# Columns of the near scores kept by place within 16, and one ScalarE placement moved ahead of another, in the two units that run before the main loop

## The chip, the core and the metric

The kernel runs on one core of a Trainium2 chip. The metric is the device time of one execution, in microseconds. Five engines work side by side and wait for each other on semaphores: TensorE (PE, with its weight loads shown as PEld), VectorE (DVE), ScalarE (ACT), GpSimd (POOL) and SyncE (SP, which here only issues DMAs).

## What is computed

Three stages, all in float32. First a gated linear attention over 4 batches, 8 heads, 768 tokens, 48 channels, written in the reference as a recurrence:

```python
for t in range(S):
    state = alpha[:, :, t, :, None] * state + np.einsum('bhd,bhe->bhde', k[:, :, t], v[:, :, t])
    y[:, :, t] = np.einsum('bhd,bhde->bhe', q[:, :, t], state)
```

Then, on the 3072 rows of 384 numbers that this gives, a feed-forward layer `elu(x @ w_in) @ w_out` with 2048 hidden channels, and last four experts of 1024 hidden channels each, `out += p_e * (relu(x @ w1[e]) @ w2[e])`, with the probabilities `p` normalised over the experts.

## The kernel before

Tokens are taken in 12 units of 256. The feed-forward and expert layers go over 6 tiles of 512 tokens in 48 steps each; every float32 product there is made of three products of rounded parts (`hi` and `lo`), so a step is 18 matmuls of 128x512. Attention for units 2 to 11 is cut into pieces that run between the steps of the tile before. Attention for units 0 and 1 (`EARLY` chunks of 128 tokens, four of them) has nothing to run beside: it stands ahead of the loop over steps, and the change touches only this part.

**Scores by levels.** Within a chunk of 128 tokens the decayed scores between tokens are made by doubling. At level `l`, with span `h = 2**l`, tokens pair up in blocks of `2h`: the queries of the right half of each block meet the keys of the left half. PE makes those scores (`early_pairs`), then DVE multiplies the right queries and left keys by their decays (`early_updates`, lines 701 and 702: the products of decays are doubled at line 710), and the next level can begin. So PE and DVE take turns within a unit, and the two units are interleaved by `EARLY_ORDER`: (unit, level) = (0,0) (0,1) (0,2) (1,0) (0,3) (1,1) (0,4) (1,2) (0,5) (1,3) (0,6) (1,4) (1,5) (1,6).

**Levels 0 to 5** are made by `early_pairs` with 64 matmuls of 64 keys by 32 right queries (line 481), keys of 64 tokens against the 32 queries of those tokens which stand to the right at this level. Every level thus gives whole 64x32 blocks, of which only some places are wanted. **Level 6** uses `level` (line 445), 32 matmuls of 64x64.

**Placing the scores.** For the spans 1, 2, 4 and 8 (`l < MASKED`) DVE copies under a mask from PSUM into `near`, a piece of the buffer `blocks` with 64 columns for each head and half (`early_masked`, line 725, two instructions a level, 256 elements each). For spans 16 and 32 the wanted places are rectangles, and ACT copies them one by one (`early_rect`, line 917: 8 copies of 16x128, or 4 of 32x256). Then ACT copies `near` into the weights of the unit (`early_near`, line 926: 2 copies of 64x1024; the weights of unit 0 are `pair_weights`, those of unit 1 stand in `p_rows`). Span 64 goes from PSUM to the weights directly (`early_rect` at level 6, line 908: 4 copies of 64x256).

**After the levels** PE turns the keys (`transpose_k`, line 500), ACT brings them to SBUF (`k_tokens`, line 933, `k_tok`), PE multiplies them with the values (`outer`, line 518), DVE adds that to the state (line 744), and `attend` (lines 542, 546, 551) gives the output of each chunk, which ACT (`x_hi`, line 959) and DVE (`x_lo`, line 756) bring to SBUF as the input of the first step. All orders are written out by hand. The lists of PE and of ACT in this part:

```python
for u, l in EARLY_ORDER[:-2]: early_pairs(u, l)
transpose_k(0); transpose_k(1); early_pairs(1, LEVELS - 2); outer(0); early_pairs(1, LEVELS - 1)
attend(0); transpose_k(2); transpose_k(3); attend(1); outer(1); attend(2); attend(3)
```

```python
early_rect(0, MASKED); early_rect(0, MASKED + 1); early_near(0)
early_rect(1, MASKED); early_rect(0, LEVELS - 1); k_tokens(0); k_tokens(1)
early_rect(1, MASKED + 1); early_near(1); early_rect(1, LEVELS - 1); k_tokens(2); k_tokens(3)
```

`outer(0)` waits for span 64 of unit 0 and, by chunk, for `k_tokens`. `attend(0)` waits for `early_near(0)`.

Of the kernel before, what the change touches and what calls it, by code (L numbers as in the profile page):

```python
# [11 lines left out]
B, HEADS, S, D = 4, 8, 768, 48  # L12
P = 128
# [3 lines left out]
HALF = P // 2  # L17
TOKENS = B * S
LEVELS = 7
LOW = 4  # L20
SUB = 1 << LOW
COL = 32
# [23 lines left out]
LEAD = 2  # L46
EARLY = 2 * LEAD
MASKED = 4
PARTS = 10

NPROD = SUB - 1
# [97 lines left out]
def program(nc, q_d, k_d, a_d, v_d, qb_d, kb_d, ab_d, k0_d, v0_d, w_d, probs_d, eye_d, masks_d, sc_d, pn_d, out):  # L149
    ctx = ExitStack()  # L150
    with ctx:
# [12 lines left out]
        QT = sbs("q_low", 2, [P, PAIRS, UNIT])  # L164
# [254 lines left out]
        def _(pe):  # L419
# [38 lines left out]
            def early_pairs(u, l):  # L458
# [15 lines left out]
                for c in range(2):  # L474
                    for pr in range(PAIRS):
                        for j in range(2):
                            t = slice(P * c + HALF * j, P * c + HALF * (j + 1))
                            for sd in range(2):
                                r = slice(HALF * sd, HALF * (sd + 1))
                                right = QT[u][r, pr, t].rearrange("p (n two h) -> p n two h", two=2, h=1 << l)[:, :, 1, :]  # L480
                                last = nc.tensor.matmul(banks[sd][HALF * j:HALF * (j + 1), COL * (PAIRS * c + pr):COL * (PAIRS * c + pr + 1)],  # L481
                                                        KL[u][r, pr, t], right, start=True, stop=True)
                last.then_inc(e_step[u], 1)
# [167 lines left out]
        def _(dve):  # L651
# [60 lines left out]
            def early_masked(u, l):  # L712

                h = 1 << l
                dve.wait_ge(e_step[u], l + 1)
                if l:
                    dve.wait_ge(e_mask[u], l)
                else:
                    dve.wait_ge(masks_in, 16)
                    dve.wait_ge(near_clear, 1)  # L720
                mask = mk[:, l, :].rearrange("p (n h) -> p n h", h=h).unsqueeze(1).broadcast_to([P, HEADS, COL // h, h])
                for sd in range(2):
                    dst = near[:, u].rearrange("p (a s) (n two h) -> p s a n two h", s=2, two=2, h=h)[:, sd, :, :, 1, :]
                    src = ps_l[l % 2][u][sd][:, 0:HEADS * COL].rearrange("p (a n h) -> p a n h", a=HEADS, h=h)
                    last = nc.vector.copy_predicated(dst, mask.bitcast(U32), src)
                last.then_inc(e_mask[u], 1)

# [153 lines left out]
        def _(act):  # L881
# [18 lines left out]
            def early_rect(u, l):  # L900
# [8 lines left out]
                else:  # L909
                    if l == MASKED:  # L910
                        act.wait_ge(e_mask[u], MASKED)
                    for sd in range(2):
                        dst = near[:, u].rearrange("p (a s) t -> p s a t", s=2)[:, sd]
                        src = ps_l[l % 2][u][sd][:, 0:HEADS * COL].rearrange("p (a t) -> p a t", a=HEADS)
                        for m in range(HALF // h):
                            rows, n = slice(2 * m * h, (2 * m + 1) * h), m % (COL // h)
                            last = nc.scalar.copy(dst[rows, :, (2 * n + 1) * h:(2 * n + 2) * h], src[rows, :, n * h:(n + 1) * h])
                last.then_inc(e_rect[u], 1)

            def early_near(u):  # L920
                act.wait_ge(e_rect[u], LEVELS - 1 - MASKED)
                act.wait_ge(cleared, CLEARS)
                w = weights[u].rearrange("p c a t -> p (c a) t")
                for m in range(2):
                    rows = slice(HALF * m, HALF * (m + 1))
                    last = nc.scalar.copy(w[rows, :, rows], near[rows, u])
                last.then_inc(e_near, 1)

            def k_tokens(g):
# [72 lines left out]
            early_rect(0, MASKED)  # L1002
            early_rect(0, MASKED + 1)
            early_near(0)
            early_rect(1, MASKED)
            early_rect(0, LEVELS - 1)
            k_tokens(0)
            k_tokens(1)
            early_rect(1, MASKED + 1)
# [204 lines left out]
```

## Time and profile before

| | before |
|---|---|
| time, median of 3 runs | 1322.0 us (1321.72 to 1322.02) |
| profiled execution | 1323.48 us, of which the span from first to last instruction is 1321.5 us |
| PE busy | 1303.8 us, 99% of the span |
| DVE, ACT, POOL busy | 64%, 46%, 40% |
| granted TensorE clock | 1.0 in every slice |

Busy shares here are for the whole span. The changed part is the first 52 us of it, and what it is worth is read there, from the instructions in order of time. A matmul's end is modelled, and matmuls overlap, so a group of matmuls starts some 0.2 us before the modelled end of the group ahead. A duration is followed in some rows by the idle time of that engine before it, and by what ended this.

### The profile page before, as it was taken

The numbers are of one execution on the slowest core, as the hardware profiler recorded it, in microseconds if no ns is written. First come the engines' busy times: TensorE is split into PE (matmuls) and PEld (weight loads), VectorE is DVE, ScalarE is ACT, GpSimd is POOL, SyncE is SP. The second block draws the span as 40 slices with busy tenths as digits, with TensorE's granted clock in tenths as the row PEclk, the third lists the DMA queues.
The fourth block names the chain that finished last, engine by engine and source line by source line (L and its number), as shares of the span: only waits on it lengthen the run. The fifth ranks groups of instructions, "written<-read, shape, count | busy, mean of one in ns | idle before, by whom it ended". The sixth has DMA issues, their size and how long they took to land.

```text
span 1321.5 us, 26259 instructions
## 1 busy us (share of the span) xinstructions
PE 1303.8 (99%) x10472; PEld 1074.5 (81%) x10472; DVE 846.1 (64%) x1129; ACT 607.8 (46%) x1051; POOL 532.6 (40%) x454
## 2 busy tenths in 40 slices
PE   6999999999999999999999999999999999999999
PEld 6787888888888888888888888888888888888887
DVE  7786767665676665576766567676557645654455
ACT  3656443357434347534336743434753433663332
POOL 1571858711655841453861175583145311100011
PEclk9999999999999999999999999999999999999999
DMA  5535353355244236336336534423623332533330
GB/s 199 177 104 174 107 185 93 96 153 186 89 137 151 76 101 198 126 108 200 89 87 169 171 91 150 144 85 93 215 98 109 100 97 87 151 96 99 101 93 31
DMA packets 84028, 165.77 MB, mean 125 GB/s; under 512 B 30146, under 2 KB 31683, under 8 KB 83908
## 3 DMA queue, kind: packets, MB, share of 16 engines
q1 hardware_dynamic: 83616, 163.97, 40.1%
q8 instruction: 83, 1.36, 0.4%
q14 instruction: 37, 0.30, 0.1%
q10 hardware_dynamic: 292, 0.13, 0.0%
HBM read 157.99 MB, written 6.08 MB: 124 GB/s over the span
## 4 chain that ended last, share of the span: by engine, by line
PE 93%; DVE 4%; ACT 2%; issue 1%; DMA 0%; ACTq 0%; DVEq 0%
PE ps_o L573 15%; PE ps_h L573 14%; PE ps_o L574 14%; PE ps_o L575 14%; PE ps_h L574 14%; PE ps_h L575 14%; PE ps_att L445 2%; DVE w_lo L749 1%; PE ps_att L542 1%; PE ps_att L518 1%; DVE elu_out L762 1%; PE ps_att L481 1%; PE ps_att L546 1%; PE ps_att L500 1%; PE ps_att L551 1%
## 5 line engine op out<-in xcount | busy, mean ns | idle before, releaser
L749 DVE TENSOR_TENSOR w_lo<-w_stage,w_hi 128x768 fp32r<-128x768 f32 x288 | 336.2, 1168 | 30.8 <-ACT w_hi L948 27.2
L573 PE MATMUL ps_o<-g_hi,w_lo 128*128 128x512 f32 x864 | 342.5, 396 | 1.5 <-DVE g_lo L766 1.5
L573 PE MATMUL ps_h<-x_hi,w_lo 128*128 128x512 f32 x864 | 337.7, 391 | 2.4 <-DVE x_lo L756 1.3
L574 PE MATMUL ps_o<-g_lo,w_hi 128*128 128x512 f32 x864 | 336.7, 390 | 0.0
L575 PE MATMUL ps_o<-g_hi,w_hi 128*128 128x512 f32 x864 | 336.6, 390 | 0.0
L574 PE MATMUL ps_h<-x_lo,w_hi 128*128 128x512 f32 x864 | 336.4, 389 | 0.0
L575 PE MATMUL ps_h<-x_hi,w_hi 128*128 128x512 f32 x864 | 336.2, 389 | 0.0
L979 ACT ACTIVATE g_hi<-ps_h 128x512 fp32r<-128x512 f32 x184 | 110.0, 598 | 476.1 <-PE ps_h L575 476.1
L770 DVE SCALAR_TENSOR_TENSOR g_lo<-ps_h,g_hi 128x512 fp32r<-128x512 f32 x184 | 126.9, 690 | 249.1 <-ACT g_hi L979 248.8
L948 ACT CAST w_hi<-w_stage 128x768 fp32r<-128x768 f32 x288 | 239.4, 832 | 13.8 <-DMA w_stage<-in_w 12.7
L280 POOL TENSOR_TENSOR products<-blocks 128x384 f32<-128x384 f32 x150 | 195.8, 1320 | 86.8 <-DVE scores L685 81.0
L573 PEld LDWEIGHTS ps_h<-x_hi,w_lo 128*128 128x128 f32 x864 | 162.2, 188 | 40.4 <-issue 3.8
L573 PEld LDWEIGHTS ps_o<-g_hi,w_lo 128*128 128x128 f32 x864 | 162.1, 188 | 37.6 <-DVE g_lo L766 2.3
L1131 POOL TENSOR_TENSOR acc<-acc,part 128x512 f32<-128x512 f32 x51 | 73.5, 1469 | 292.4 <-DVE part L810 292.4
L575 PEld LDWEIGHTS ps_o<-g_hi,w_hi 128*128 128x128 f32 x864 | 162.2, 188 | 34.1
L575 PEld LDWEIGHTS ps_h<-x_hi,w_hi 128*128 128x128 f32 x864 | 162.2, 188 | 33.8
L574 PEld LDWEIGHTS ps_h<-x_lo,w_hi 128*128 128x128 f32 x864 | 162.2, 188 | 33.3
L574 PEld LDWEIGHTS ps_o<-g_lo,w_hi 128*128 128x128 f32 x864 | 162.3, 188 | 32.0
L1111 POOL TENSOR_TENSOR k_level<-k_level,decay 128x512 f32<-128x512 f32 x30 | 36.3, 1208 | 230.7 <-PE ps_att L445 230.7
L766 DVE TENSOR_TENSOR g_lo<-elu_out,g_hi 128x512 fp32r<-128x512 f32 x104 | 77.2, 743 | 66.6 <-ACT g_hi L974 61.1
L762 DVE SCALAR_TENSOR_TENSOR elu_out<-elu_exp,ps_h 128x512 f32<-128x512 f32 x96 | 65.9, 686 | 65.2 <-ACT elu_exp L968 65.2
L974 ACT CAST g_hi<-elu_out 128x512 fp32r<-128x512 f32 x96 | 59.6, 621 | 94.9 <-DVE elu_out L762 61.0
(103 smaller groups left out, 1017.3 us busy)
## 6 DMA issues: line engine op xcount, KB each, us to landing
w_stage<-in_w SPq DMA_DIRECT2D x288, 384.0 KB, 3.1
k_level<-in_k SPq DMA_DIRECT2D x12, 512.0 KB, 5.8
q_low<-in_q SPq DMA_DIRECT2D x12, 512.0 KB, 6.5
alpha<-in_a SPq DMA_DIRECT2D x12, 512.0 KB, 4.2
v_tok<-in_v SPq DMA_DIRECT2D x12, 512.0 KB, 4.6
p_rows<-p_norm SPq DMA_DIRECT2D x6, 1024.0 KB, 9.2
out<-acc SPq DMA_DIRECT2D x18, 256.0 KB, 4.3
blocks<-in_q_blocks SPq DMA_DIRECT2D x10, 384.0 KB, 3.9
```

Source lines behind the costliest of these rows:

```text
L280: return engine.tensor_tensor(dst, q[:, :, 1, i:i + 1, :].broadcast_to([P, pairs, h, D]), k[:, :, 0], ALU.mult)
L573: nc.tensor.matmul(dst, lhs[1], rhs[0], start=first, stop=False)
L574: nc.tensor.matmul(dst, lhs[0], rhs[1], start=False, stop=False)
L575: return nc.tensor.matmul(dst, lhs[0], rhs[0], start=False, stop=last)
L749: nc.vector.tensor_tensor(wl[n % WRING][:], stage[n % STAGE][:], wh[n % WRING][:].bitcast(F32), ALU.subtract).then_inc(w_low, 1)
L762: nc.vector.scalar_tensor_tensor(gt[n % 2][:], ex[n % 2][:], -1.0, ps_h[n % 2][:], ALU.add, ALU.max).then_inc(h_read, 1)
L766: nc.vector.tensor_tensor(gl[n % GS][:], gt[n % 2][:], gh[n % GS][:].bitcast(F32), ALU.subtract).then_inc(g_ready, 1)
L770: nc.vector.scalar_tensor_tensor(gl[n % GS][:], ps_h[n % 2][:], 0.0, gh[n % GS][:].bitcast(F32), ALU.max, ALU.subtract).then_inc(g_ready, 1)
L948: nc.scalar.copy(wh[n % WRING][:], stage[n % STAGE][:]).then_inc(w_hi, 1)
L974: nc.scalar.copy(gh[n % GS][:], gt[n % 2][:]).then_inc(g_hi, 1)
L979: nc.scalar.activation(gh[n % GS][:], ps_h[n % 2][:], ACT.Relu).then_inc(g_hi, 1)
L1131: nc.gpsimd.tensor_tensor(acc[:, m, :], acc[:, m, :], part[k % 2][:], ALU.add).then_inc(acc_added, 1)
```

## The change

It has two parts. First, the 64 columns of `near`, and for levels 0 to 3 also the 32 columns of the scores in PSUM, stand in another order: with `INNER` = 16 and `OUTER` = 4, a token of 64 at place `z` within its 16, in the `w`-th 16, has column `4*z + w` (before: `16*w + z`). For `l < MASKED` PE writes the columns in the new order by reading the queries in it. For spans 16 and 32 PE's order stays, and ACT's copy writes to columns 4 apart. `early_near` puts the columns back: it reads them 4 apart and writes them side by side. The masks are made in the new order by the host. Second, in ACT's list the placing of span 64 of unit 0 stands ahead of span 16 of unit 1 instead of behind it. The core of the diff:

```diff
+INNER = 1 << MASKED
+OUTER = HALF // INNER
...
-                                right = QT[u][r, pr, t].rearrange("p (n two h) -> p n two h", two=2, h=1 << l)[:, :, 1, :]
+                                if l < MASKED:
+                                    right = QT[u][r, pr, t].rearrange("p (w n two h) -> p n two h w", w=OUTER, two=2, h=1 << l)[:, :, 1]
+                                else:
+                                    right = QT[u][r, pr, t].rearrange("p (n two h) -> p n two h", two=2, h=1 << l)[:, :, 1, :]
...
-                mask = mk[:, l, :].rearrange("p (n h) -> p n h", h=h).unsqueeze(1).broadcast_to([P, HEADS, COL // h, h])
+                mask = mk[:, l, :].rearrange("p (n x) -> p n x", x=OUTER * h).unsqueeze(1).broadcast_to([P, HEADS, INNER // 2 // h, OUTER * h])
...
-                    dst = near[:, u].rearrange("p (a s) (n two h) -> p s a n two h", s=2, two=2, h=h)[:, sd, :, :, 1, :]
-                    src = ps_l[l % 2][u][sd][:, 0:HEADS * COL].rearrange("p (a n h) -> p a n h", a=HEADS, h=h)
+                    dst = near[:, u].rearrange("p (a s) (n two x) -> p s a n two x", s=2, two=2, x=OUTER * h)[:, sd, :, :, 1, :]
+                    src = ps_l[l % 2][u][sd][:, 0:HEADS * COL].rearrange("p (a n x) -> p a n x", a=HEADS, x=OUTER * h)
...
-                        dst = near[:, u].rearrange("p (a s) t -> p s a t", s=2)[:, sd]
-                        src = ps_l[l % 2][u][sd][:, 0:HEADS * COL].rearrange("p (a t) -> p a t", a=HEADS)
+                        dst = near[:, u].rearrange("p (a s) (z w) -> p s a w z", s=2, z=INNER)[:, sd]
+                        src = ps_l[l % 2][u][sd][:, 0:HEADS * COL].rearrange("p (a w z) -> p a w z", a=HEADS, z=INNER)
...
-                    last = nc.scalar.copy(w[rows, :, rows], near[rows, u])
+                    last = nc.scalar.copy(w[rows, :, rows].rearrange("p a (w z) -> p a w z", z=INNER),
+                                          near[rows, u].rearrange("p a (z w) -> p a w z", z=INNER))
...
             early_near(0)
+            early_rect(0, LEVELS - 1)
             early_rect(1, MASKED)
-            early_rect(0, LEVELS - 1)
             k_tokens(0)
...
-    near = np.arange(HALF)
+    near = np.arange(HALF).reshape(OUTER, INNER).T.reshape(HALF)
```

ACT's list around the moved step, before. `near` stands in `blocks`; `ps_att2` and `ps_o0` hold span 16 of unit 1, `ps_att0` and `ps_att1` span 64 of unit 0:

```order
L926 COPY pair_weights<-blocks 64x16x64
L917 COPY blocks<-ps_att2 16x8x16 [waits early_pairs_masked_1,early_pairs_done_1]
L917 COPY blocks<-ps_att2 16x8x16 x3
L917 COPY blocks<-ps_o0 16x8x16 x4
L908 COPY pair_weights<-ps_att0 64x2x2x64 [waits cleared,early_pairs_done_0]
L908 COPY pair_weights<-ps_att0 64x2x2x64
L908 COPY pair_weights<-ps_att1 64x2x2x64 x2
L933 COPY k_tok_0<-ps_h0 128x512 [waits k_transposed]
```

The same place after:

```order
L932 COPY pair_weights<-blocks 64x16x64
L913 COPY pair_weights<-ps_att0 64x2x2x64 [waits cleared,early_pairs_done_0]
L913 COPY pair_weights<-ps_att0 64x2x2x64
L913 COPY pair_weights<-ps_att1 64x2x2x64 x2
L923 COPY blocks<-ps_att2 16x8x16 [waits early_pairs_masked_1,early_pairs_done_1]
L923 COPY blocks<-ps_att2 16x8x16 x3
L923 COPY blocks<-ps_o0 16x8x16 x4
L940 COPY k_tok_0<-ps_h0 128x512 [waits k_transposed]
```

The four copies of span 64 now stand ahead of the eight of span 16, and the copies of the keys behind both, as before.

DVE's list from level 0 of unit 1 to level 1 of unit 1, before. `decay_0` and `decay_1` belong to the units 0 and 1; the numbers of the masked copies are partitions, heads and the runs of the pattern:

```order
L725 COPY_PREDICATED blocks<-masks,ps_att 128x8x32
L725 COPY_PREDICATED blocks<-masks,ps_o 128x8x32
L701 TENSOR_TENSOR q_low<-q_low,decay_0 128x64x8
L702 TENSOR_TENSOR k_level<-k_level,decay_0 128x64x8
L710 TENSOR_TENSOR decay_0<-decay_0 128x64
L725 COPY_PREDICATED blocks<-masks,ps_h 128x8x4x8 x2
L701 TENSOR_TENSOR q_low<-q_low,decay_1 128x256x2
L702 TENSOR_TENSOR k_level<-k_level,decay_1 128x256x2
L710 TENSOR_TENSOR decay_1<-decay_1 128x256
L725 COPY_PREDICATED blocks<-masks,ps_o 128x8x16x2 x2
L701 TENSOR_TENSOR q_low<-q_low,decay_0 128x32x16
```

After:

```order
L730 COPY_PREDICATED blocks<-masks,ps_att 128x8x8x4
L730 COPY_PREDICATED blocks<-masks,ps_o 128x8x8x4
L706 TENSOR_TENSOR q_low<-q_low,decay_0 128x64x8
L707 TENSOR_TENSOR k_level<-k_level,decay_0 128x64x8
L715 TENSOR_TENSOR decay_0<-decay_0 128x64
L730 COPY_PREDICATED blocks<-masks,ps_h 128x8x32 x2
L706 TENSOR_TENSOR q_low<-q_low,decay_1 128x256x2
L707 TENSOR_TENSOR k_level<-k_level,decay_1 128x256x2
L715 TENSOR_TENSOR decay_1<-decay_1 128x256
L730 COPY_PREDICATED blocks<-masks,ps_o 128x8x4x8 x2
L706 TENSOR_TENSOR q_low<-q_low,decay_0 128x32x16
```

The order is the same; the runs of the masked copies at spans 1, 2, 4 and 8 are 4, 8, 16 and 32 elements long, where they were 1, 2, 4 and 8. PE's list has the same instructions in the same order.

## Rows read from the trace of the kernel before

**Rows 1.** Busy by engine in stretches: start:end, length, PE, PEld, DVE, ACT, POOL, clock, DMA.

```profile
35.00:40.00 5.00, 4.46 (x134) 3.93 (x132) 3.59 (x7) 4.82 (x16) 0.69 (x1) 1.00 0.36 105
60.00:1321.00 1261.00, 1257.11 (x9237) 1032.33 (x9237) 800.50 (x1043) 580.50 (x995) 515.86 (x435) 1.00 0.40 123
```

**Rows 2.** DVE in order of time: start, duration, instructions, idle before.

```profile
12.06 0.69 DVE L701 TENSOR_TENSOR q_low<-q_low,decay 128x512 f32<-128x512 f32 x1 [0.30 <-PE ps_h L481]
...
22.98 0.69 DVE L701 TENSOR_TENSOR q_low<-q_low,decay 128x512 f32<-128x512 f32 x1 [0.23 <-PE ps_o L481]
...
24.53 1.29 DVE L725 COPY_PREDICATED blocks<-masks,ps_o 128x256 f32<-128x256 uint32 x2
25.61 0.73 DVE L701 TENSOR_TENSOR q_low<-q_low,decay 128x512 f32<-128x512 f32 x1
26.25 0.68 DVE L702 TENSOR_TENSOR k_level<-k_level,decay 128x512 f32<-128x512 f32 x1
...
32.17 0.76 DVE L725 COPY_PREDICATED blocks<-masks,ps_o 128x256 f32<-128x256 uint32 x2
32.83 0.69 DVE L701 TENSOR_TENSOR q_low<-q_low,decay 128x512 f32<-128x512 f32 x1
...
39.04 0.68 DVE L702 TENSOR_TENSOR k_level<-k_level,decay 128x512 f32<-128x512 f32 x1
```

**Rows 3.** The chain that ended last: start, duration, what.

```profile
19.97 1.39 issue
...
26.73 0.30 issue
...
28.96 1.71 PE ps_o L481 x64
...
37.90 0.59 ACT k_tok L933
```

**Rows 4.** ACT in order of time, from span 32 of unit 0 on.

```profile
29.02 1.49 ACT L917 COPY blocks<-ps_h 32x256 f32<-32x256 f32 x4 [2.29 <-PE ps_h L481]
30.53 2.10 ACT L926 COPY pair_weights<-blocks 64x1024 f32<-64x1024 f32 x2
34.21 1.06 ACT L917 COPY blocks<-ps_att 16x128 f32<-16x128 f32 x4 [1.58 <-PE ps_o L481]
35.28 1.06 ACT L917 COPY blocks<-ps_o 16x128 f32<-16x128 f32 x4
36.37 1.51 ACT L908 COPY pair_weights<-ps_att 64x256 f32<-64x256 f32 x4
37.90 1.07 ACT L933 COPY k_tok<-ps_h 128x512 f32<-128x512 f32 x2
...
44.54 1.07 ACT L933 COPY k_tok<-ps_o 128x512 f32<-128x512 f32 x2 [0.54 <-PE ps_o L500]
```

**Rows 5.** PE in order of time, from level 5 of unit 1 to `outer(1)`.

```profile
36.34 1.93 PE L481 MATMUL ps_o<-q_low,k_level 64*64 64x32 f32 x64 [0.18 <-issue]
38.63 1.51 PE L518 MATMUL ps_att<-v_tok,k_tok 128*32 128x48 f32 x64 [0.36 <-ACT k_tok L933]
40.07 0.37 PE L445 MATMUL ps_att<-q_low,k_level 64*64 64x64 f32 x1
...
41.13 0.65 PE L542 MATMUL ps_h<-q_low,state 128*32 128x128 f32 x8
...
44.87 0.43 PE L542 MATMUL ps_h<-q_low,state 128*32 128x128 f32 x8
...
46.42 0.86 PE L518 MATMUL ps_att<-v_tok,k_tok 128*32 128x48 f32 x64
```

**Rows 6.** Four groups on DVE by form, in 0 to 120: busy us, mean ns, idle.

```profile
L685 DVE TENSOR_REDUCE scores<-products 128x8 f32<-128x384 f32 x15 | 7.8, 546 | 0.0
...
L710 DVE TENSOR_TENSOR decay<-alpha 128x512 f32<-128x512 f32 x2 | 1.4, 684 | 0.0
...
L710 DVE TENSOR_TENSOR decay<-decay 128x256 f32<-128x256 f32 x2 | 0.8, 419 | 0.0
...
L814 DVE TENSOR_REDUCE p_sum<-p_raw 128x24 f32<-128x96 f32 x1 | 0.3, 320 | 0.0
```

More of the change, by code:

```diff
@@ L912, in early_rect @@
                     for sd in range(2):
-                        dst = near[:, u].rearrange("p (a s) t -> p s a t", s=2)[:, sd]
-                        src = ps_l[l % 2][u][sd][:, 0:HEADS * COL].rearrange("p (a t) -> p a t", a=HEADS)
+                        dst = near[:, u].rearrange("p (a s) (z w) -> p s a w z", s=2, z=INNER)[:, sd]
+                        src = ps_l[l % 2][u][sd][:, 0:HEADS * COL].rearrange("p (a w z) -> p a w z", a=HEADS, z=INNER)
+                        wide = h // INNER
                         for m in range(HALF // h):
                             rows, n = slice(2 * m * h, (2 * m + 1) * h), m % (COL // h)
-                            last = nc.scalar.copy(dst[rows, :, (2 * n + 1) * h:(2 * n + 2) * h], src[rows, :, n * h:(n + 1) * h])
+                            last = nc.scalar.copy(dst[rows, :, (2 * n + 1) * wide:(2 * n + 2) * wide], src[rows, :, n * wide:(n + 1) * wide])
                 last.then_inc(e_rect[u], 1)
```

## The prediction

> **What bounds the kernel now.** The busy time by stretches comes first: from 60 us on PE is busy for 1257.11 of 1261 us [rows 1]. Nothing of the change stands there, and whatever the first part gains or loses should shift this stage as a whole. So I read only the first 52 us, engine by engine in order of time, beside the chain that ended last. Two things are to be seen. Up to 34 us PE and DVE take turns: DVE's idle time before a query update is 0.30 us at 12.06 and 0.23 us at 22.98, and each ends with PE [rows 2], while PE in its turn waits 0.30 us at 26.73 [rows 3] for a key update of DVE that ends at 26.25 + 0.68 = 26.93 [rows 2]. From 34.21 to 38.49 (37.90 + 0.59 [rows 3]) ACT works without a pause through span 16 of unit 1, span 64 of unit 0 and the first copy of the keys, and PE's `outer(0)` waits for the end of that, 0.36 us [rows 4, 5]. ACT's share in 35 to 40 is 4.82 of 5 us [rows 1].
>
> **Masked copies on DVE.** With runs of 2 elements (24.53) a pair takes 1.29 us and the next instruction starts 25.61 - 24.53 = 1.08 us after the pair; with runs of 8 (32.17) these are 0.76 and 32.83 - 32.17 = 0.66 us [rows 2]. The change gives every pair runs of 4 or more. I take the 0.66 of runs of 8 for all, so each of the four pairs at spans 1 and 2 saves 0.42 us, 1.7 us of DVE together; the bounds are 0 and this. What of it lies on the path: behind the span-1 pair of unit 0 DVE waits for PE anyway (0.30 us at 12.06), and behind span 2 too, since PE's level takes 1.71 us [rows 3] and starts only with the key update. So nothing there. The span-1 pair of unit 1 ends before DVE waits for PE at 22.98 [rows 2], and PE was late then by a stall of 1.39 us at 19.97 that has no releaser in the profile [rows 3]; this I leave where it is, and the 0.42 us becomes idle time. The span-2 pair of unit 1, at 24.53, is followed without a pause by the updates for which PE waits at 26.73. They come 0.42 us earlier, but PE has its own work until 26.73, so level 5 of unit 0 starts at 26.75 instead of 27.03: **0.28 us** on the path. From there on PE, DVE and ACT pass this on by level, and level 5 of unit 1 starts at 36.34 - 0.28 = 36.06 on PE [rows 5].
>
> **Span 64 moved in ACT's list.** It needs level 6 of unit 0, which PE makes before level 4 of unit 1, and ACT was idle for 1.58 us before 34.21, waiting for that level 4 [rows 4]. The four copies take 1.51 us [rows 4], which fits. With span 32 starting at 29.02 - 0.28 = 28.74, ACT has 1.49 and 2.10 us to 32.33, the moved 1.51 us to 33.84, waits to 34.21 - 0.28 = 33.93, has 2.14 us for span 16 to 36.07, and with 0.59 us [rows 3] the first `k_tok` ends at 36.66, the second at 37.14 [rows 4]. They were at 38.49 and 38.97 (37.90 + 1.07). The keys are turned by then, since PE does it ahead of level 5. Nothing that is moved past waits on more than before: no DMA is issued there, and the copies of the keys keep their place behind both.
>
> Who is late next: PE itself. Level 5 of unit 1 starts at 36.06 and holds PE for 1.71 us [rows 3], to 37.77, where `outer(0)` started at 38.63 [rows 5]: 0.86 us earlier. It takes 40.07 - 38.63 = 1.44 us [rows 5], to 39.21. But level 6 of unit 1 also needs DVE's key update of level 5, which ended at 39.04 + 0.68 = 39.72 [rows 2] and follows PE's level 5, so it ends at 39.44; with the 0.1 us that such a handover takes (26.93 to 27.03), level 6 starts at 39.54 instead of 40.07. So of 1.79 us that ACT is earlier, **0.53 us** in all, with the 0.28 in it, reach the path. Behind it stand `attend(0)`, the turned keys of unit 1 and `attend(1)`; ACT had 0.54 us to spare before the next copy of the keys, at 44.54 [rows 4], and keeps it.
>
> **A price at PE's speed.** The profile grants PE a clock of 1.00 in each of these stretches [rows 1], yet the same 8 matmuls of `attend` last 0.65 us at 41.13 and 0.43 us at 44.87 [rows 5]; by that they run at 1.2 GHz before about 44.9 us and at 2.4 GHz after. If the step stays at its time, 0.53 us of the faster work is now done slowly, and the gain falls to some 0.27 us; if it moves with the work, it stays 0.53. I take 0.5.
>
> **Strides, the unknown cost.** Three accesses change from side by side to apart: ACT writes `near` 16 bytes apart at spans 16 and 32, ACT reads `near` 16 bytes apart in `early_near`, and PE reads its queries 64 bytes apart at levels 0 to 3. No ACT or PE instruction of the trace does that. The lower bound is no cost, since the number of elements stays. The upper bound is from the nearest row, DVE's reduction of `p_raw`, which reads 96 elements each 96 bytes apart in 320 ns. Elements side by side cost (684 - 419) / 256 = 1.035 ns [rows 6], the long reduction's fixed part is then 546 - 384 x 1.035 = 149 ns, and the strided element costs (320 - 149) / 96 = 1.78 ns. ACT's own rate is (0.3725 - 0.265) / 128 = 0.84 ns, from a copy of 256 and one of 128 elements [rows 4]. The value that I take is no cost, by a small margin: DVE's query update at span 2 (12.06), which reads and writes 8 of every 16 bytes, takes the same 0.69 us as the one at span 64 (32.83) [rows 2], and 16 bytes apart is nearer to that than to 96. But it is no proof.
>
> The Trainium skill, "Advanced Engine Details and Errata", section "SBUF Cachelines", speaks against this change: a line of SBUF is 16 bytes, and an access pattern with fewer than two hits on a line pays. It gives no figure. The reduction above agrees with it, and the update at span 2, with two hits on a line, does not speak against it. By this rule the result would be the first rival; by the row of the update alone it would be my sum.
>
> **Rival 1, ACT slower on both sides.** At 1.78 instead of 0.84 ns an element, span 16 costs 8 x 128 x 0.94 ns = 0.96 us more, span 32 4 x 256 x 0.94 = 0.96 and `early_near` 2 x 1024 x 0.94 = 1.93: 3.85 us a unit. ACT from 28.74: span 32 to 31.19, `early_near` to 35.22, span 64 to 36.73, span 16 to 39.83, `k_tok` to 40.42, and `outer(0)` starts at 40.56, 1.9 us late. Then the second `k_tok` to 40.90, span 32 of unit 1 to 43.35, `early_near(1)` to 47.38, its span 64 to 48.89, the third `k_tok` to 49.48, and `outer(1)` starts at 49.6 instead of 46.42 [rows 5]: 3.2 us slower, **1325.2 us**. It decides from the point at which ACT's chain, 42.74 at the third `k_tok` without any extra, passes 46.28: an extra of 46% of 7.7 us, or 1.27 ns an element. From 1.59 ns on the loss is over 0.2%.
>
> **Rival 2, one side only.** If only writes or only reads suffer, the extra is half, 3.85 us, and `outer(1)` starts 0.2 us late: **1322.1 us**, no change.
>
> **Rival 3, PE slower on its strided queries.** 32 matmuls of level 6 with 64 columns start within 41.13 - 40.07 = 1.06 us, 33.1 ns each [rows 5], 64 with 32 columns in 1.71 us, 26.7 ns each [rows 3]. So 32 columns are worth 6.4 ns, and at half the rate a level takes 0.41 us more. Eight levels are 3.3 us at most; if the stall at 19.97 swallows what is lost ahead of it, only what follows counts, two levels and two thirds of one, 1.1 us. With the 0.5 gained this gives 1322.6 to 1324.8, middle **1323.6 us**. For it: two tiles of columns read at once. Against it: PE wants a column only every 0.8 ns and each in turn.
>
> **Rival 4, PE's speed rises earlier.** The pause before `outer(0)` goes, and PE is busy without one from earlier on. Nothing in the rows says at what time the rise would then come; I put it at 41.6, one microsecond into the new `attend(0)` (from 40.60). `attend(0)` and the turned keys took from 41.13 to 44.87, 3.74 us [rows 5]; the 2.7 us of it that remain go in 1.4, and with the 0.5 of the sum the first step starts 1.8 us earlier: **1320.2 us**. Against it: the pause does not vanish, it moves behind `outer(0)` (39.21 to 39.54).
>
> **Rival 5, the masked copies don't get faster.** Then `outer(0)` starts at 38.05, and level 6 is held by a key update that ends at 39.72, so it starts at 39.82: 0.25 us, **1321.8 us**.
>
> **The numbers.** The profiled execution took 1323.48 us with a span of 1321.5; the median is 1322.0, and the difference of 1.5 us is the profiler's. The forecast is a span of 1321.0, and 1322.0 - 0.5 = 1321.5 us. Chances: forecast 0.36, rival 1 0.25, rival 2 0.15, rival 3 0.12, rival 4 0.09, rival 5 0.03. 0.2% is 2.6 us, about what a measurement of this kernel can tell from no change. Faster by more: 0.02, the end of rival 4. Slower by more: 0.20 of rival 1 and 0.04 of rival 3. Within: 0.74. The range goes from 1320.0 (rival 4) to 1325.4 (rival 1); outside stay some 0.02 below and 0.10 above.
>
> **What would show it.** Masked copies of 0.43 us at all spans; ACT's `early_near` copies at 1.04 us each (rival 1: near 2.0) and the rectangles at 0.26 and 0.36 us (0.38 and 0.60); span 64 of unit 0 in ACT's list at about 32.3; level 5 of unit 0 on PE at 26.75; `outer(0)` at 37.8, level 6 at 39.5; 64 matmuls of a level in 1.71 us still (rival 3: 2.1). Wrong would be made of any strided copy that takes longer, a stall like that at 19.97 in another place, or a chain that has gained in ACT's list but not in the start of `outer(0)`.

## The result, and the profile after

The changed kernel takes 1326.24 us (median of 8 executions, 1325.61 to 1328.61) against 1322.01 us (8 executions, 1321.45 to 1323.21): a ratio of 1.0033, with a 95% interval of 1.0025 to 1.0042. It is 4.2 us slower. The forecast was 1321.5, and the time is also above the range, which ended at 1325.4.

The masked copies did become as fast as forecast. Line 730 of the changed kernel is line 725 of before, 923 is 917, 932 is 926. By source line (duration in ns as min/median/max, then first and last start):

```profile
L730 DVE COPY_PREDICATED blocks<-masks,ps_att x6: 425/430/450, 10.2 to 27.4; 128x256 f32<-128x256 uint32 x6
...
L923 ACT COPY blocks<-ps_att x12: 373/388/397, 24.1 to 37.5; 16x128 f32<-16x128 f32 x12
...
L923 ACT COPY blocks<-ps_h x4: 614/632/642, 28.0 to 30.0; 32x256 f32<-32x256 f32 x4
...
L932 ACT COPY pair_weights<-blocks x2: 2052/2058/2065, 30.6 to 32.7; 64x1024 f32<-64x1024 f32 x2
```

Every span now has 0.43 us, where spans 1 and 2 took 1.29 us a pair [rows 2]. But each ACT copy of the near scores takes longer: 0.388 us instead of 0.265, 0.632 instead of 0.372, and 2.06 instead of 1.05 [rows 4; there a group's duration divided by its count]. ACT's list in order of time, in the changed kernel:

```profile
28.04 2.56 ACT L923 COPY blocks<-ps_h 32x256 f32<-32x256 f32 x4 [0.78 <-PE ps_h L486]
30.62 4.13 ACT L932 COPY pair_weights<-blocks 64x1024 f32<-64x1024 f32 x2
34.78 1.51 ACT L913 COPY pair_weights<-ps_att 64x256 f32<-64x256 f32 x4
36.31 1.55 ACT L923 COPY blocks<-ps_att 16x128 f32<-16x128 f32 x4
37.87 1.53 ACT L923 COPY blocks<-ps_o 16x128 f32<-16x128 f32 x4
39.43 1.07 ACT L940 COPY k_tok<-ps_h 128x512 f32<-128x512 f32 x2
40.39 2.48 ACT L923 COPY blocks<-ps_o 32x256 f32<-32x256 f32 x4
42.90 4.21 ACT L932 COPY p_rows<-blocks 64x1024 f32<-64x1024 f32 x2
...
48.67 1.07 ACT L940 COPY k_tok<-ps_o 128x512 f32<-128x512 f32 x2
```

From 28.04 to 50 us ACT has no idle time at all. The moved step (34.78) no longer fills a gap, since there is none. PE in order of time shows who waits for that: `outer(0)` 2.87 us and `outer(1)` 0.65 us, both for a copy of the keys on ACT, and the first step of the main part starts at 54.83.

```profile
40.16 1.51 PE L523 MATMUL ps_att<-v_tok,k_tok 128*32 128x48 f32 x64 [2.87 <-ACT k_tok L940]
...
49.40 0.94 PE L523 MATMUL ps_att<-v_tok,k_tok 128*32 128x48 f32 x64 [0.65 <-ACT k_tok L940]
...
54.83 0.47 PE L578 MATMUL ps_h<-x_hi,w_lo 128*128 128x512 f32 x1 [1.27 <-DVE x_lo L761]
```

In the kernel before these three stood at 38.63, 46.42 [rows 5] and 51.89:

```profile
51.89 0.47 PE L573 MATMUL ps_h<-x_hi,w_lo 128*128 128x512 f32 x1 [1.27 <-DVE x_lo L756]
```

What follows the first step is the same. In the trace of before it is 1321.5 - 51.89 = 1269.6 us long, in the changed kernel's 1324.1 - 54.83 = 1269.3. So the loss lies wholly ahead of it: 2.94 us between these two traces, and 4.2 between the medians. That the two differ needs an explanation of its own, and the experiments give it.

### The profile page after: what moved, and what is told of

Same layout as the page of the kernel before. It is cut to its first block, busy times and chain, and to the rows that moved or that the text cites. A ratio compares the mean times of both kernels' runs of the same rounds, so it can differ in the third digit from the quotient of the medians.

```text
span 1324.1 us, 26259 instructions
## 1 busy us (share of the span) xinstructions
PE 1304.2 (98%) x10472; PEld 1074.5 (81%) x10472; DVE 844.1 (64%) x1129; ACT 615.9 (47%) x1051; POOL 532.1 (40%) x454
## 4 chain that ended last, share of the span: by engine, by line
PE 92%; DVE 4%; ACT 2%; issue 2%; DMA 0%; ACTq 0%; DVEq 0%
PE ps_o L578 15%; PE ps_h L578 14%; PE ps_o L580 14%; PE ps_o L579 14%; PE ps_h L580 14%; PE ps_h L579 14%; PE ps_att L447 2%; DVE w_lo L754 1%; PE ps_att L547 1%; DVE elu_out L767 1%; PE ps_att L523 1%; PE ps_att L505 1%; PE ps_att L551 1%; PE ps_att L556 1%; ACT g_hi L981 1%
```

## The experiments

Two theories stood against each other at first. By the main one, ACT's copies of columns 16 bytes apart carry the loss, through the two waits of PE for `k_tok`. By its rivals something else of the change costs time: the moved step, PE's strided queries, or the speed of PE. Each comparison below is with executions of the kernel before on the same chip.

### One part of the change at a time

**The move alone**, on the kernel before:

```diff
             early_near(0)
+            early_rect(0, LEVELS - 1)
             early_rect(1, MASKED)
-            early_rect(0, LEVELS - 1)
```

> The kernel before with the second part of the change alone: span 64 of unit 0 is placed ahead of span 16 of unit 1 in ScalarE's list. Main theory (ScalarE's copies 16 bytes apart are the whole loss): none is here, so outer(0) starts at about 38.05 where TensorE comes free instead of 38.63, level 6 at 39.8, and the time is 1321.8 us, 0.2 to 0.3 below before. Rival (the moved step itself costs, since it delays span 16 of unit 1 or shifts TensorE's change of speed): slower than before, up to 1 us.

Measured: 1322.49 us against 1322.64, ratio 0.9996 (0.9987 to 1.0005). In its trace `outer(0)` starts at 38.18 (38.05 expected) and level 6 of unit 1 at 39.80, as expected, and the moved step stands in the gap at 32.64:

```profile
30.51 2.10 ACT L926 COPY pair_weights<-blocks 64x1024 f32<-64x1024 f32 x2
32.64 1.50 ACT L908 COPY pair_weights<-ps_att 64x256 f32<-64x256 f32 x4
34.18 1.06 ACT L917 COPY blocks<-ps_att 16x128 f32<-16x128 f32 x4
```

So the move does what it says and does not cost; its 0.2 us can't be told from nothing.

**The layout alone**, the changed kernel with the moved step put back:

```diff
             early_near(0)
-            early_rect(0, LEVELS - 1)
             early_rect(1, MASKED)
+            early_rect(0, LEVELS - 1)
```

> The changed kernel with the moved step put back. Main theory: with early_near at 4.1 us ScalarE has no idle time left before span 16 of unit 1, so the order of the two steps is worth nothing: first k_tok ends at the same time as in the changed kernel (about 40.0), 1326.2 us. Rival (the moved step costs): 1325 us or less.

Measured: 1326.66 us, ratio 1.0031 (1.0019 to 1.0042), the loss of the whole change. The rival that blamed the moved step has fallen.

**The layout without ACT's share.** The rectangles are written side by side and `early_near` copies side by side. The masked places still stand in the new order, so the weights near the diagonal come out in a wrong order of columns; the instructions and their sizes stay:

```diff
-                        dst = near[:, u].rearrange("p (a s) (z w) -> p s a w z", s=2, z=INNER)[:, sd]
+                        dst = near[:, u].rearrange("p (a s) (w z) -> p s a w z", s=2, z=INNER)[:, sd]
...
-                    last = nc.scalar.copy(w[rows, :, rows].rearrange("p a (w z) -> p a w z", z=INNER),
-                                          near[rows, u].rearrange("p a (z w) -> p a w z", z=INNER))
+                    last = nc.scalar.copy(w[rows, :, rows], near[rows, u])
```

> The changed kernel with all of ScalarE's copies side by side again (the columns of the weights near the diagonal stand in the wrong order for it): masked copies on VectorE, TensorE's queries 64 bytes apart and the moved step stay. Main theory: 0.5 us faster than before, 1321.5, early_near 1.04 us a copy, outer(0) at 37.8. Rival (TensorE's strided queries, or a later change of its speed, cost the part of the loss that the ScalarE sum does not give, some 1.2 us): 1323 or more.

Measured: 1322.23 us against 1322.64, ratio 0.9998 (0.9989 to 1.0006). The loss is gone, with PE's queries still 64 bytes apart. The 0.5 us of gain that was expected can't be told from nothing in this interval. Its `early_near` takes 2.10 us for two copies again:

```profile
29.47 2.10 ACT L932 COPY pair_weights<-blocks 64x1024 f32<-64x1024 f32 x2
```

### Reads, writes and distances

**Only the writes apart** (`early_near` as in the last diff, the rectangles as in the changed kernel), and **only the reads apart** (the other way round). Both, too, leave columns in a wrong order:

> The changed kernel with ScalarE's writes of spans 16 and 32 kept 4 columns apart, but early_near copying side by side (columns come out in the wrong order). Main theory (cost adds up on ScalarE's list until it is late for outer(1)): rectangles 0.38 and 0.62 us, early_near 1.04, outer(0) at about 38.1, outer(1) not late, 1321.5 us, within 0.5. Rival (every microsecond of extra ScalarE work is a microsecond of the kernel): half of the loss, 1324.

> The changed kernel with the rectangles written side by side, but early_near reading 4 columns apart (wrong order of columns). Main theory: early_near 2.05 to 2.1 us a copy, outer(0) at about 38.05, outer(1) at 46.3 to 46.7, 1322.1 us, within 0.3 of before. Rival as above: 1324.

Measured: 1323.02 us, ratio 1.0006 (0.9997 to 1.0015), and 1323.40 us, ratio 1.0008 (0.9999 to 1.0017), both against 1322.31. Half of ACT's extra time gives 0.7 and 1.1 us. Neither can be told from nothing, as both intervals hold 1, though both medians lie above the 1321.5 and 1322.1 expected. The traces show why it is so little: PE does wait for ACT before `outer(0)`, 1.28 and 0.74 us, but the group starts at 38.28 and 38.51, not later than the 38.63 of the trace of before. The third copy of the keys starts at 44.67 with the writes apart, so that PE does not wait before `outer(1)` (46.49), and at 46.06 with the reads apart, where PE waits 1.28 us and `outer(1)` starts at 46.79.

```profile
38.28 1.51 PE L523 MATMUL ps_att<-v_tok,k_tok 128*32 128x48 f32 x64 [1.28 <-ACT k_tok L939]
...
44.67 1.07 ACT L939 COPY k_tok<-ps_o 128x512 f32<-128x512 f32 x2
```

```profile
29.91 4.16 ACT L932 COPY pair_weights<-blocks 64x1024 f32<-64x1024 f32 x2
...
46.06 1.07 ACT L940 COPY k_tok<-ps_o 128x512 f32<-128x512 f32 x2
...
46.79 0.94 PE L523 MATMUL ps_att<-v_tok,k_tok 128*32 128x48 f32 x64 [1.28 <-ACT k_tok L940]
```

The first fence is the one with writes apart, the second the one with reads apart; each has lines of PE's list and of ACT's. The two costs add up on ACT's list, and the kernel pays only what passes the point at which PE wants the keys. That is why half of the extra costs less than half of the 4.2 us.

**`early_near` the other way.** It reads side by side and writes 64 bytes apart:

```diff
-                    last = nc.scalar.copy(w[rows, :, rows].rearrange("p a (w z) -> p a w z", z=INNER),
-                                          near[rows, u].rearrange("p a (z w) -> p a w z", z=INNER))
+                    last = nc.scalar.copy(w[rows, :, rows].rearrange("p a (w z) -> p a z w", z=INNER),
+                                          near[rows, u].rearrange("p a (z w) -> p a z w", z=INNER))
```

> The changed kernel with early_near going through the columns in the other order: it reads side by side and writes 64 bytes apart, the result is the reference's. Main theory (a copy pays once per element when either side has one element to a 16-byte line): 2.05 us a copy, 1326.2 us as the changed kernel. Rival (only reads pay in this copy, writes less): 1.6 us a copy and about 1324.

Measured: 1325.96 us, ratio 1.0026 (1.0016 to 1.0036), and 3.92 us for the two copies instead of 4.13:

```profile
30.46 3.92 ACT L932 COPY pair_weights<-blocks 64x1024 f32<-64x1024 f32 x2
```

A write 64 bytes apart costs nearly what a read 16 bytes apart costs, and turning the loop round moves the price to the other side.

**Eight bytes instead of sixteen.** The same idea with two groups of 32 places:

```diff
-INNER = 1 << MASKED
-OUTER = HALF // INNER
+OUTER = 2
+INNER = HALF // OUTER
...
-                        src = ps_l[l % 2][u][sd][:, 0:HEADS * COL].rearrange("p (a w z) -> p a w z", a=HEADS, z=INNER)
-                        wide = h // INNER
+                        src = ps_l[l % 2][u][sd][:, 0:HEADS * COL].rearrange("p (a t) -> p a t", a=HEADS)
...
-                            last = nc.scalar.copy(dst[rows, :, (2 * n + 1) * wide:(2 * n + 2) * wide], src[rows, :, n * wide:(n + 1) * wide])
+                            w, z = divmod((2 * n + 1) * h, INNER)
+                            last = nc.scalar.copy(dst[rows, :, w, z:z + h], src[rows, :, n * h:(n + 1) * h])
```

> The changed layout with places within 32 instead of 16, so that columns stand 8 bytes apart for ScalarE and masked copies have runs of 2, 4, 8 and 16. If ScalarE pays only from 16 bytes on: early_near 1.04 us a copy, rectangles 0.26 and 0.36, span-1 masked copies 0.75 us and all others 0.43, the pair on the path is among the fast ones, so 1321.5 us, 0.5 below before. If any distance costs (rival): early_near near 2.05 us and about 1326.

Measured: 1322.51 us against 1322.64, ratio 0.9998 (0.9989 to 1.0007). ACT in order of time:

```profile
27.79 1.56 ACT L923 COPY blocks<-ps_h 32x256 f32<-32x256 f32 x4 [1.77 <-PE ps_h L486]
29.39 2.28 ACT L932 COPY pair_weights<-blocks 64x1024 f32<-64x1024 f32 x2
```

The step lies between 8 and 16 bytes: 1.14 us a copy against 1.05 side by side and 2.06 at 16 bytes. On DVE the span-2 pair (runs of 4) takes 0.76 us and the span-1 pair (runs of 2) 1.31:

```profile
9.98 1.31 DVE L730 COPY_PREDICATED blocks<-masks,ps_att 128x256 f32<-128x256 uint32 x2
13.13 0.76 DVE L730 COPY_PREDICATED blocks<-masks,ps_h 128x256 f32<-128x256 uint32 x2
```

This version keeps half of the gain on DVE and loses little on ACT (0.18 us for the two copies of `early_near`), and still its median can't be told from before. No run here gives a version that beats the kernel before.

### Why 4.2 and not 3.2: the speed of PE

The sum of the first rival gave 3.2 us. To see what the last microsecond was, the changed kernel was run once more for a second trace, and the kernel before twice.

> The changed kernel on the chip of the three runs above, for its spread and a second trace. Main theory: ScalarE's extra gives outer(1) at 49.4 in any trace, 1325.6 to 1326.5; what is above in single runs is TensorE's change of speed coming later, behind attend(1). Rival: something that no trace has shown costs a further microsecond in all runs.

Measured: 1326.64 us, single executions 1326.04 to 1328.05, against 1322.31; the ratio is 1.0032 (1.0020 to 1.0044). The traced execution is the slowest, 1328.05 us, and its stretches (columns as in rows 1, the clock third from the end) hold records of the clock:

```profile
38.00:42.00 4.00, 1.58 (x68) 1.49 (x72) 0.77 (x4) 3.90 (x10) 0.00 (x0) 0.50 0.07 27
...
46.00:50.00 4.00, 2.16 (x84) 1.76 (x85) 0.59 (x1) 3.92 (x8) 1.28 (x1) 1.00 0.27 74
50.00:54.00 4.00, 4.00 (x128) 3.94 (x120) 1.73 (x4) 1.19 (x4) 2.23 (x2) 0.62 0.91 307
```

A clock of 0.50 is 1.2 GHz. PE's instructions in order of time, same trace:

```profile
49.74 0.94 PE L523 MATMUL ps_att<-v_tok,k_tok 128*32 128x48 f32 x64 [1.84 <-ACT k_tok L940]
50.64 0.43 PE L547 MATMUL ps_o<-q_low,state 128*32 128x128 f32 x8
50.85 0.63 PE L551 MATMUL ps_o<-p_rows,v_tok 128*32 128x128 f32 x8
51.19 0.72 PE L547 MATMUL ps_o<-q_low,state 128*32 128x128 f32 x8
...
56.84 0.47 PE L578 MATMUL ps_h<-x_hi,w_lo 128*128 128x512 f32 x1 [1.27 <-DVE x_lo L761]
```

PE had paused for 1.84 us ahead of `outer(1)`, and at about 51 us it fell back to 1.2 GHz. From `outer(1)` to the first step it took 7.10 us here and 5.43 in the first trace. A plainer fallback stands in the trace of the layout alone: PE was at the faster rate, paused for 4.54 us, and came back at the slower one (its clock reads 0.50 in 38 to 42 us):

```profile
34.32 1.14 PE L486 MATMUL ps_o<-q_low,k_level 64*64 64x32 f32 x64 [0.22 <-issue]
40.00 1.51 PE L523 MATMUL ps_att<-v_tok,k_tok 128*32 128x48 f32 x64 [4.54 <-ACT k_tok L940]
```

> The kernel before, unchanged, for a second trace. Theory S (before's single runs differ because TensorE's change from 1.2 to 2.4 GHz falls at another time within attend(0) to attend(3)): the first step starts at another time than 51.89 us, between 50 and 52.5, and the time of this execution is about 1271.4 us more than that start (1269.5 of main part and 1.9 around the span); everything behind the first step is as long as in the first trace. Rival (the difference arises in the main part): first step at 51.9 whatever the time.

> As the look before it, a third trace of the kernel before: the time minus the start of the first step is 1271.4 again, within 0.4 (theory S), or the start of the first step is the same and the rest differs (rival).

Measured: 1323.12 and 1322.14 us. With the other traces of the same kinds, all starts from PE in order of time:

| trace | `outer(0)` | `outer(1)` | first step | time | time minus first step |
|---|---|---|---|---|---|
| before | 38.63 | 46.42 | 51.89 | 1323.48 | 1271.6 |
| before, second | 38.57 | 46.31 | 51.73 | 1323.12 | 1271.4 |
| before, third | 38.31 | 44.63 | 51.12 | 1322.14 | 1271.0 |
| move alone | 38.18 | 45.16 | 51.21 | 1322.62 | 1271.4 |
| ACT side by side | 37.14 | 44.12 | 50.25 | 1321.27 | 1271.0 |
| eight bytes | 36.17 | 43.10 | 49.14 | 1320.24 | 1271.1 |
| changed | 40.16 | 49.40 | 54.83 | 1326.20 | 1271.4 |
| changed, again | 40.42 | 49.74 | 56.84 | 1328.05 | 1271.2 |

Theory S holds for the most part: in these eight traces an execution's time is the start of its first step and 1271.0 to 1271.6 us. In the other eight the difference is 1270.8 (ACT's copies twice, below) to 1272.0 (1326.86 - 54.88, short fillings), so up to 1.2 us of a difference between two executions can lie behind the first step. Within one kernel the start of the first step differs with the time at which PE goes from 1.2 to 2.4 GHz. In the third trace of before level 5 of unit 1 is already at the faster rate:

```profile
36.03 1.14 PE L481 MATMUL ps_o<-q_low,k_level 64*64 64x32 f32 x64 [0.27 <-issue]
...
44.63 0.86 PE L518 MATMUL ps_att<-v_tok,k_tok 128*32 128x48 f32 x64
...
46.80 0.31 PE L546 MATMUL ps_o<-p_rows,v_tok 128*32 128x128 f32 x3 [0.69 <-issue]
...
51.12 0.47 PE L573 MATMUL ps_h<-x_hi,w_lo 128*128 128x512 f32 x1 [1.27 <-DVE x_lo L756]
```

In the first trace it took 1.93 us at 36.34, and the rate was still the slow one in `attend(0)` at 41.13 [rows 5]. Not all of what the faster rate gives reaches the first step: `outer(1)` is 1.79 us earlier in the third trace than in the first, the first step 0.77. In between PE stands still for 0.69 us that the profile gives no releaser for, which the first trace does not show.

The trace I predicted from was thus a late one: 1323.48 us lies at the upper end of the executions of before. The profiler adds no fixed time: in the thirteen other kernels and repeats whose traced execution is among the timed ones, it lies between 2.3 us below and 1.4 us above the median, and 0.1 below on average. With 1271.4 for what follows, the median of 1322.0 belongs to a first step at 1322.0 - 1271.4 = 50.6. The changed kernel can't use an early change, because `outer(1)` waits for ACT and starts at 49.30 to 49.74 in four traces (changed, changed again, the layout alone, short fillings), though PE goes to the faster rate at different times in them. Its 54.83 minus 50.6 is 4.2 us again, but that only says the medians over once more, since both starts are a time less 1271.4. The comparison that needs no median is the one with the third trace, whose 1322.14 us is close to it: the changed kernel's `outer(1)` starts 4.77 us later, its first step 3.71, and its time is 4.06 longer, where the first trace gave 2.98, 2.94 and 2.72.

### Filling PE's pauses, and giving ACT the same time without strides

**Two fillings on the kernel before**, behind levels 0 and 1 of unit 0, and **two on the changed kernel**, ahead of `outer(0)` and `outer(1)`, by matmuls that nobody reads:

```diff
+                    nc.tensor.matmul(bank[:, at:at + P], eye[:], eye[:], start=True, stop=True)
...
+                if (u, l) in ((0, 0), (0, 1)):
+                    pe.wait_ge(eye_in, 16)
+                    fill(ps_o[2], 2 * P, 5)
```

```diff
+            pe.wait_ge(e_rect[0], LEVELS - MASKED)
+            fill(ps_a[0], 3 * P, 9)
             outer(0)
...
+            fill(ps_a[0], 3 * P, 9)
             outer(1)
```

> The kernel before with five matmuls of 128x128 that nobody reads behind each of levels 0 and 1 of unit 0, where TensorE waits 1.5 us for VectorE, so that it has no pause from 6 to 17 us. Theory S with the step set by earlier busy time: the change to 2.4 GHz comes at 10 to 20 us instead of 38 to 45, levels take about 1.0 us instead of 1.9, and what VectorE and ScalarE let through is 1 to 3 us faster, 1319.5 to 1321.5. Rival (the step comes when it comes, or TensorE falls back at the next pause): same as before, or up to 0.3 slower.

> The changed kernel with nine matmuls that nobody reads in each of the two pauses that TensorE has ahead of outer(0) and outer(1), 2.9 and 0.7 to 1.8 us long. Theory: the pauses let TensorE fall back to 1.2 GHz in some runs, which costs the last attends up to 1.7 us; filled, the runs above 1327 are gone, but outer(1) still waits for ScalarE at 49.4 and the time is 1325.6 to 1326.3. Rival (the pauses have no part in the spread): as the changed kernel, 1325.6 to 1328.6. If the loss came from TensorE's speed and not from ScalarE: 1324 or less.

Measured: 1323.45 us, ratio 1.0010 (1.0001 to 1.0019), and 1330.16 us, ratio 1.0063 (1.0049 to 1.0077), against 1321.78. Both outlasted the pauses, since each such matmul is two instructions and takes 0.5 us at the slower rate, not the 0.24 that I had taken from the transposing ones:

```profile
12.73 2.50 PE L617 MATMUL ps_o<-eye 128*128 128x128 f32 x10
15.16 2.02 PE L481 MATMUL ps_att<-q_low,k_level 64*64 64x32 f32 x65
18.66 1.93 PE L481 MATMUL ps_h<-q_low,k_level 64*64 64x32 f32 x64
```

The first still says something. PE is busy for the whole of 12 to 20 us in this trace of the filled kernel, and a level takes 1.93 us at 18.66 as in the kernel before. Earlier busy time alone did not bring the faster rate, and that expectation has fallen. The second told nothing of its question. It is 3.9 us slower than the changed kernel. Its `outer(1)` starts at 50.78, 1.4 us later, and the rest is a standstill of 2.58 us without a releaser in the last `attend`, behind which PE is again at the slower rate (the first matmul of the first step takes 0.77 us instead of 0.47):

```profile
57.30 0.63 PE L556 MATMUL ps_o<-p_rows,v_tok 128*32 128x128 f32 x12 [2.58 <-issue]
```

It was done again with short fillings, three and two:

```diff
+            fill(ps_a[0], 3 * P, 3)
             outer(0)
...
+            fill(ps_a[0], 3 * P, 2)
             outer(1)
```

> The changed kernel with shorter fillings than before: three matmuls of 128x128 ahead of outer(0) and two ahead of outer(1), some 1.5 and 0.5 us, so that neither outlasts the pause. Theory: outer(0) stays at about 40.2 and outer(1) at 49.4, TensorE no longer falls back to 1.2 GHz behind outer(1), and the runs above 1327 are gone: 1325.6 to 1326.5. Rival (fallback does not depend on these pauses): 1325.6 to 1328.6 as the changed kernel.

Measured: 1326.86 us, five executions from 1326.69 to 1326.92, against 1322.25; ratio 1.0036 (1.0023 to 1.0048). The spread is 0.2 us where the changed kernel's fourteen executions spread over 3.0, and none of the five is near 1328. But the median is above the 1326.5 expected at most and above both medians of the changed kernel, so the fillings gained nothing on the whole. The loss stays, since `outer(1)` still waits for ACT:

```profile
46.53 0.71 PE L622 MATMUL ps_att<-eye 128*128 128x128 f32 x4
49.44 0.94 PE L523 MATMUL ps_att<-v_tok,k_tok 128*32 128x48 f32 x64 [2.20 <-ACT k_tok L947]
```

Five executions without one near 1328 fit the theory that the pauses cause the fallback; they do not prove it. In this trace pauses of 2.81 and 2.20 us are left, ahead of `outer(0)` and `outer(1)`, and PE's rate did not fall behind either.

**ACT's time alone**, on the kernel before, with each copy of span 32 and of `early_near` also made to a spare place:

```diff
+                            if l > MASKED:
+                                nc.scalar.copy(spare[u][rows, 1024 + 256 * sd:1280 + 256 * sd].rearrange("p (a t) -> p a t", a=HEADS), src[rows, :, n * h:(n + 1) * h])
...
+                    nc.scalar.copy(spare[u][rows, 0:1024].rearrange("p (a t) -> p a t", a=2 * HEADS), near[rows, u])
                     last = nc.scalar.copy(w[rows, :, rows], near[rows, u])
```

> The kernel before with its layout and order, but ScalarE does the copies of span 32 and of early_near twice, the second time to a place that nobody reads: 7.2 us more on its list, as much as the strided copies add in the changed kernel, and no access apart. Theory (only ScalarE's time counts, since outer(0) and outer(1) wait for it): outer(0) at 41.0, outer(1) at about 50.3 in its trace, 1326.5 to 1327.5 us. Rival (the wider accesses also slow something else, or TensorE's speed is the cause): 1325 or less.

Measured: 1325.77 us against 1322.25, ratio 1.0028 (1.0017 to 1.0038), 3.5 us slower, between the 1326.5 of the theory and the 1325 of its rival. `outer(1)` starts at 48.71, not 50.3, as the added copies overlap with their neighbours (4 pairs of span 32 end 2.55 us after the first starts, not 2.98):

```profile
48.71 0.94 PE L518 MATMUL ps_att<-v_tok,k_tok 128*32 128x48 f32 x64 [0.98 <-ACT k_tok L938]
```

No access is apart in this kernel, and the layout and order are those of before. So time on ACT's list alone brings a loss of this kind. Its `outer(1)` starts 0.69 us before the changed kernel's, and its median lies 0.5 us below, which agrees: nothing else of the change is needed.

## Why the prediction was wrong

**What bounds the first part**: right. PE waits for ACT's `k_tok`, and behind the first step nothing changes (1269.3 and 1269.6 us).

**Masked copies on DVE**: the price was right, 0.76 us a pair at every span. What reaches the path was sized too low. Level 5 of unit 1 starts 29.88 us after level 0 in the trace of before (36.34 - 6.46) and 29.15 after it in the changed kernel's (35.35 - 6.20), 0.73 us less instead of 0.28. Of this, 0.28 lie in PE's stall at 19.97, which is 1.11 us instead of 1.39:

```profile
19.71 1.11 issue
20.82 1.38 PE ps_o L486 x42
```

This part can't be put down to the change: from level 0 to the stall's end it is 14.63 to 15.00 us in five traces with the layout of before and 14.35 to 14.95 in ten with a new one. The rest can. Level 5 of unit 0 starts 5.67 or 5.68 us behind the stall's end in each of the five, 5.22 or 5.23 in each of the ten:

```profile
27.03 1.93 PE L481 MATMUL ps_h<-q_low,k_level 64*64 64x32 f32 x64 [0.30 <-issue]
```

```profile
26.05 1.94 PE L486 MATMUL ps_h<-q_low,k_level 64*64 64x32 f32 x64 [0.18 <-issue]
```

So 0.44 us, the whole saving of the span-2 pair (0.42 reckoned), reaches the path. I had let PE's own work hold it until 26.73; in the changed kernel that work ends at 25.86, and level 5 waits for DVE alone (its key update ends at 25.94).

**Span 64 moved**: right by itself (the run with the move alone gave 38.18 and 39.80 for 38.05 and 39.8), and worth nothing in the changed kernel, where ACT has no gap to fill.

**Strides, the unknown cost**: this is the step that failed. I took no cost "by a small margin", from DVE's update at span 2, an instruction on another engine that reads 8 of every 16 bytes. An element 16 bytes apart costs ACT (0.64 - 0.3875) / 128 = 1.97 ns instead of 0.84, from the copies of 256 and 128 elements (2.56 / 4 and 1.55 / 4 us). The nearest row in kind was the other one, the reduction with one element to each 16-byte line and 1.78 ns, and the rule of the Trainium skill ("Advanced Engine Details and Errata", section "SBUF Cachelines") said the same. The runs agree with it on ACT: two elements on a line cost 1.14 us a copy, one on a line 2.06. Row and rule together should have made rival 1 the forecast. For PE's moving operand the rule did not show: the levels at spans 4 and 8 of unit 0, 64 bytes apart, take 1.99 and 2.00 us, to the digit what they take in the trace of before. All these levels ran at the slower rate, so nothing is shown for the faster one:

```profile
13.19 1.99 PE L486 MATMUL ps_att<-q_low,k_level 64*64 64x32 f32 x65 [1.55 <-DVE q_low L706]
17.07 2.00 PE L486 MATMUL ps_h<-q_low,k_level 64*64 64x32 f32 x64
```

**Rival 1** was the right mechanism with nearly the right places: `outer(0)` at 40.56 reckoned and 40.16 found, `outer(1)` at 49.6 and 49.40. Its time of 1325.2 was a microsecond short for a second reason, the step that put the time beyond the range: I took the 1.5 us between the profiled execution and the median for the profiler's, a constant. It was a late execution. A good half of its distance to the third trace (0.77 of 1.34 us) is PE's change of speed and what hangs on it, ahead of the first step; what the other 0.6, behind it, are stays open. A wait that ends at a fixed time has to be measured against the first step that goes with the median (50.6 by the estimate above), not against the trace's (51.89). Its threshold holds a slip as well: only 49.48 - 42.74 = 6.74 of the 7.7 us stand ahead of the third `k_tok`, so `outer(1)` is late from 53% of the extra on, 1.33 ns an element, and not from 46% and 1.27. The measured 1.97 is past both.

**Rivals 2 to 5**: one side only gives 0.7 and 1.1 us, where 0.1 was reckoned. The intervals do not tell these from nothing; if they are real, it is the same error of base, as `outer(1)` at 46.49 or 46.79 is level with the late trace of before but not with its third (44.63). PE's strided queries cost nothing at the slower rate. The masked copies did get faster. PE's earlier change, which I gave 0.09, is found in the third trace of before and in those of the move alone, of ACT side by side and of eight bytes: it is an ordinary state of affairs of this kernel, not an effect of the change. The gain of 0.5 us that the forecast was built on was never told from nothing: with ACT side by side, the case that it describes, the median is 0.4 below before and the interval holds 1.

## What to carry to other kernels

A permuted layout moves its cost to whoever undoes it: count both ends, and ask for each engine how many elements of an access share 16 bytes. On ACT one float32 to each 16 bytes doubled a copy of 1024 elements, two cost 9%. Before taking one trace as the base, see where its time lies among the other executions, and find the wait whose end moves from one to the next; a change that turns such a floating wait into a fixed one loses more than a late trace shows.

## What was not expected of the hardware

The granted clock stands at 1.00 in the first 32 us of all sixteen traces, although a level takes 1.93 us there and 1.14 at the full rate. Lower values appear in five of them only, and each time as a fall from 1.00 behind 32 us (the layout alone, only writes apart, the changed kernel again and with long fillings, ACT's copies twice). In three of these (only writes apart, the changed kernel again, ACT's copies twice) PE had gone to the faster rate at about 30 us, where level 4 of unit 1 takes 0.22 us a matmul instead of 0.29, and fell between 33 and 35, when it had been without a matmul for 0.86 us; the rise itself left no mark in the clock. So the rate is better read from the duration of one form (0.65 and 0.43 us for 8 matmuls of 128x128). With PE busy without a pause from 12 to 20 us the rate stayed at 1.2 GHz, while the kernel before changed at 44.9 us in one trace and before 36.03 in another. What sets that moment stays open; in the three traces of before it moves `outer(1)` by up to 1.8 us, and single executions of before lie up to 3 us apart. On DVE a masked copy of 256 float32 starts its successor after 0.33 us with runs of 4 or more and after some 0.54 with runs of 1 or 2, while plain updates of the same runs show no such step.
